# Gated linear attention and two expert layers: warming products, the key-value product and the two highest score levels moved

## The reference

```python
for t in range(S):                      # 4 batches x 8 heads, S = 768, head_dim 48
    state = alpha[:, :, t, :, None] * state + np.einsum('bhd,bhe->bhde', k[:, :, t], v[:, :, t])
    y[:, :, t] = np.einsum('bhd,bhde->bhe', q[:, :, t], state)
...
for e in range(E):                      # x is y as 3072 x 384; 4 experts of 384 x 1024 x 384
    h = np.maximum(x @ w1[e], 0.0)
    out += p[:, e:e + 1] * (h @ w2[e])  # p: domain_probs, normalised over the experts
...
h = x @ w_in                            # 384 x 2048 x 384
g = h * np.clip(h + 3.0, 0.0, 6.0) / 6.0
return g @ w_out
```

## Time and profile before

| | |
|---|---|
| time, median of 3 runs | 1378.64 us (1376.93 to 1380.78) |
| time of the profiled execution | 1379.01 us |
| its span | 1377.2 us |
| PE busy | 1356.5 us, 98% of the span |
| POOL, DVE, ACT busy | 57%, 49%, 39% |
| mean granted clock of TensorE | 0.98 of full |
| end of the prologue (first hidden product) | 70.68 us |

### The profile page before, as it was taken

How to read it: one execution, slowest core, us unless ns; L and a number is a source line. 1 busy time by engine, 2 the same in 40 slices (tenths; PEclk the granted TensorE clock), 3 DMA queues, 4 the chain that set the end, 5 groups by cost and what they waited for, 6 DMA issues and landing times.

```text
span 1377.2 us, 34014 instructions
## 1 busy us (share of the span) xinstructions
PE 1356.5 (98%) x13568; PEld 1107.3 (80%) x13568; DVE 678.3 (49%) x1397; ACT 534.8 (39%) x992; POOL 781.8 (57%) x865
## 2 busy tenths in 40 slices
PE   6899999999999999999999999999999999999998
PEld 5688888888888888888888888888888888888887
DVE  8776665444454544454544454454445343333333
ACT  2233333333354333354433345433335433335543
POOL 8866666655555665565656555656564444444442
PEclk6599999999999999999999999999999999999999
DMA  4243333333333433333433333343322232332331
GB/s 148 82 144 119 118 118 103 121 109 110 97 106 115 140 104 116 106 99 114 134 119 109 105 99 123 104 140 98 113 85 92 93 134 100 107 96 93 101 117 35
DMA packets 69899, 150.33 MB, mean 109 GB/s; under 512 B 8816, under 2 KB 21360, under 8 KB 69744
## 3 DMA queue, kind: packets, MB, share of 16 engines
q1 hardware_dynamic: 69744, 148.16, 34.3%
HBM read 143.36 MB, written 4.77 MB: 108 GB/s over the span
## 4 chain that ended last, share of the span: by engine, by line
PE 97%; POOL 1%; DVE 1%; issue 1%; ACT 0%; DMA 0%; DVEq 0%; POOLq 0%
PE psum L526 43%; PE psum L510 43%; PE psum L426 5%; PE psum L447 1%; PE psum L467 1%; PE psum L482 1%; PE psum L437 1%; PE psum L490 1%; POOL k_lev L906 0%; DMA alpha_q<-qa 0%; POOL decay L869 0%; DVE q_lev L595 0%; DVE psum L637 0%; POOL w_lo L925 0%; ACT x_hi L796 0%
## 5 line engine op out<-in xcount | busy, mean ns | idle before, releaser
L925 POOL TENSOR_TENSOR w_lo<-w_raw,w_hi 128x768 fp32r<-128x768 f32 (+1 forms) x291 | 531.4, 1826 | 541.8 <-ACT w_hi L815 541.8
L809 ACT ACTIVATE h_hi<-psum 128x512 fp32r<-128x512 f32 x288 | 172.3, 598 | 628.0 <-DVE psum L651 553.3
L526 PE MATMUL psum<-h_hi,w_hi 128*128 128x512 f32 x864 | 344.8, 399 | 0.2 <-DVE x_lo L673 0.2
L526 PE MATMUL psum<-h_hi,w_lo 128*128 128x512 f32 x864 | 337.2, 390 | 0.0
L526 PE MATMUL psum<-h_lo,w_hi 128*128 128x512 f32 x864 | 336.7, 390 | 0.0
L510 PE MATMUL psum<-x_hi,w_hi 128*128 128x512 f32 x864 | 336.4, 389 | 0.0
L510 PE MATMUL psum<-x_lo,w_hi 128*128 128x512 f32 x864 | 336.1, 389 | 0.0
L510 PE MATMUL psum<-x_hi,w_lo 128*128 128x512 f32 x864 | 336.0, 389 | 0.0
L651 DVE SCALAR_TENSOR_TENSOR psum<-psum,probs 128x512 f32<-128x512 f32 x192 | 134.2, 699 | 351.3 <-PE psum L510 351.2
L815 ACT ACTIVATE w_hi<-w_raw 128x768 fp32r<-128x768 f32 x288 | 241.5, 838 | 0.0
L663 DVE TENSOR_TENSOR h_lo<-psum,h_hi 128x512 fp32r<-128x512 f32 x288 | 197.7, 686 | 60.9 <-ACT h_hi L809 60.9
(11 more groups left out here) (57 smaller groups left out, 805.8 us busy)
## 6 DMA issues: line engine op xcount, KB each, us to landing
w_raw<-w SPq DMA_DIRECT2D x288, 384.0 KB, 3.1
alpha_q<-qa SPq DMA_DIRECT2D x48, 256.0 KB, 3.5
k_raw<-kk SPq DMA_DIRECT2D x48, 128.0 KB, 3.6
probs<-prob_scratch SPq DMA_DIRECT2D x24, 256.0 KB, 3.8
v_sb<-v SPq DMA_DIRECT2D x48, 96.0 KB, 2.8
out<-result SPq DMA_DIRECT2D x18, 256.0 KB, 3.9
level_sb<-level SPq DMA_DIRECT2D x1, 80.0 KB, 3.1
ident_sb<-ident SPq DMA_DIRECT2D x1, 64.0 KB, 2.8
```

The source lines that it names most:

```text
L526: mm = pe.matmul(out_bank[k], a, x[:, g % DEEP, :], start=first and i == 0, stop=last and i == 2)
L809: act.activation(h_hi[:, g % DEEP, :], h_bank[g % 2][:, :], ACT.Copy).then_inc(hh_made, 1)
L925: op = pool.tensor_tensor(w_lo[:, g % RING, cols], w_raw[:, g % RAW, cols], w_hi[:, g % RING, cols].bitcast(F32), ALU.subtract)
```

## The change

- In the prologue PE's order becomes: score(n+1), one warming product, attend(n), one warming product, turn_k(n+1), one warming product. Two more for each n from 0 to 6; around chunk 7's attend there are five and four as before.
- carry writes both halves into the chunk's own two score banks, with start=False, beside what attend wrote there. Bank 0 is left to turn_k, which now waits for `kn_made` (ACT has copied the keys of the chunk before) in place of `s_made`.
- p_kept exists twice. keep(n) step 0 and the new ACT step wait for attend(n-2) in place of attend(n-1).
- For the chunks 0 to 7, DVE's keep has four steps in place of six. The levels 5 and 4 are copied by ACT in copy_high(n+1), six instructions on 32 or 16 partitions each, placed between odd_k(n+3) and split_x(n). Step 0 becomes a predicated copy, so that it leaves ACT's parts standing, and waits for all six (`high_made`). The zeros around them are written once by POOL at the start, before its first scale_k.

```diff
+def keeps(n):
+    return KEEPS - 2 if n < PER_TILE else KEEPS
...
-        p_kept = sb("p_kept", [P, 2, 2, CH])
+        p_kept = [sb(f"p_kept{i}", [P, 2, 2, CH]) for i in range(2)]
...
 # turn_k
-                need(pe, s_made, carried(n))
+                need(pe, kn_made, carried(n))
...
 # carry
-                            lo = KV_AT + jp * HEAD_D
-                            mm = pe.matmul(kv_bank(n, jj)[own(i), lo:lo + HEAD_D], k_rows[own(jj), jp, own(i)],
-                                           v_sb[n % 2][own(jj), jp, i, :], start=jp == 0 and jj == 0, stop=True,
+                            lo = 512 * jj + KV_AT + jp * HEAD_D
+                            mm = pe.matmul(scores(n)[own(i), lo:lo + HEAD_D], k_rows[own(jj), jp, own(i)],
+                                           v_sb[n % 2][own(jj), jp, i, :], start=False, stop=True,
...
 # PE, prologue
                 keep_warm(1 if n + 1 < PER_TILE else 5)
                 attend(n)
+                keep_warm(1 if n + 1 < PER_TILE else 4)
                 if n + 1 < PER_TILE:
                     turn_k(n + 1)
-                else:
-                    keep_warm(4)
+                    keep_warm(1)
...
 # DVE, keep, step 0
-                    need(dve, y_made, n)
+                    need(dve, y_made, n - 1)
                     dve.wait_ge(p_made, n + 1)
...
+                    if n < PER_TILE:
+                        dve.wait_ge(high_made, HIGHS * (n + 1))
+                        mask = diag_sb[:, :].bitcast(I32).rearrange("p (o r m) -> p o r m", o=1, r=2)
+                        op = dve.copy_predicated(pairs, mask.to_broadcast([P, 4, 2, CH // 2]), both)
+                    else:
+                        mask = diag_sb[:, :].rearrange("p (o r m) -> p o r m", o=1, r=2)
+                        op = dve.tensor_tensor(pairs, both, mask.to_broadcast([P, 4, 2, CH // 2]), ALU.mult)
...
 # ACT
+            def copy_high(n):
...
+                need(act, y_made, n - 1)
+                act.wait_ge(p_made, n + 1)
+                for l in (LEVELS - 1, LEVELS - 2):
+                    x, at = 1 << l, CH // 2 * (l + 1)
+                    for m in range(CH // 2 // x):
+                        for jj in range(2):
+                            rows = slice(64 * jj + 2 * x * m, 64 * jj + 2 * x * m + x)
+                            act.activation(dst[rows, :, (2 * m + 1) * x:(2 * m + 2) * x],
+                                           s[rows, :, at + x * m:at + x * m + x], ACT.Copy).then_inc(high_made, 1)
...
+            copy_high(0)
             for n in range(PER_TILE):
                 copy_k_rows(n)
                 if not first_of_seq(n):
                     decay_state(n)
                 if n + 3 < K_BEFORE:
                     odd_k(n + 3)
+                if n + 1 < PER_TILE:
+                    copy_high(n + 1)
                 split_x(n)
...
 # POOL
+            for i in range(2):
+                pool.memset(p_kept[i][:, :, :, :], 0.0).then_inc(p_zeroed, 1)
```

More of the change, by code:

```diff
@@ L51 @@
 KEEPS = LEVELS
+HIGHS = 6
 K_TOP = PAIRS * CH + CH // 2
@@ L137, in last_of_seq, with kept @@
     return n % SEQ_CH == SEQ_CH - 1
+def keeps(n):
+    return KEEPS - 2 if n < PER_TILE else KEEPS
+def kept(n):
+    return sum(keeps(m) for m in range(n))
 def need(eng, sem, count):
@@ L189, in build @@
         psum = ctx.enter_context(nc.psum_tensor("psum", [P, 8 * BANK], F32))
-        state_bank = psum[:, 0:BANK]
         score_banks = psum[:, BANK:3 * BANK]
@@ L194, in build @@
         h_bank = [psum[:, i * BANK:(i + 1) * BANK] for i in (6, 7)]
-        kt_out = state_bank[:, 0:2 * P]
+        kt_out = psum[:, 0:2 * P]
         in_qa = [sem(f"in_qa{i}") for i in range(QRING)]
@@ L203, in build @@
         in_prob_rows, prob_rows_out, prob_made = sem("in_prob_rows"), sem("prob_rows_out"), sem("prob_made")
-        zeros_made, ones_made = sem("zeros_made"), sem("ones_made")
+        zeros_made, ones_made, p_zeroed = sem("zeros_made"), sem("ones_made"), sem("p_zeroed")
         three_made = sem("three_made")
@@ L210, in build @@
         pv_made, y_made = sem("pv_made"), sem("y_made")
-        keep_made, kn_made, dec_made, s_made = sem("keep_made"), sem("kn_made"), sem("dec_made"), sem("s_made")
+        keep_made, high_made, kn_made, dec_made, s_made = sem("keep_made"), sem("high_made"), sem("kn_made"), sem("dec_made"), sem("s_made")
         yt_made, x_hi_made, x_lo_made = sem("yt_made"), sem("x_hi_made"), sem("x_lo_made")
@@ L264, in scores @@
             return out_banks if n < PER_TILE and n % 2 else score_banks
-        def kv_bank(n, jj):
-            return scores(n)[:, BANK:2 * BANK] if jj else state_bank
         def kv_out(n):
-            stride = (4 if n < PER_TILE and n % 2 else 2) * BANK
-            return psum[:, 0:2 * stride].rearrange("p (a c) -> p a c", a=2)[:, :, KV_AT:KV_AT + 2 * HEAD_D].rearrange(
+            return scores(n)[:, :].rearrange("p (a c) -> p a c", a=2)[:, :, KV_AT:KV_AT + 2 * HEAD_D].rearrange(
                 "p a (b e) -> p b a e", b=2)
@@ L455, in attend @@
                 pe.wait_ge(in_v[n % 2], 16 * (n // 2 + 1))
-                pe.wait_ge(keep_made, KEEPS * (n + 1))
+                pe.wait_ge(keep_made, kept(n + 1))
                 if not last_of_seq(n):
@@ L467, in attend @@
                                 mm = pe.matmul(scores(n)[quarter(jp, x), lo:lo + HEAD_D],
-                                               p_kept[own(jj), i, jp, 32 * th:32 * th + 32],
+                                               p_kept[n % 2][own(jj), i, jp, 32 * th:32 * th + 32],
                                                v_sb[n % 2][own(jj), jp, i, :],
@@ L600, in keep @@
                 s = scores(n)[:, :].rearrange("p (a c) -> p a c", c=SLAB)
-                dst = p_kept[:, :, :, :].rearrange("p i a t -> p (i a) t")
+                dst = p_kept[n % 2][:, :, :, :].rearrange("p i a t -> p (i a) t")
                 if step == 0:
@@ L604, in keep @@
                         dve.wait_ge(in_diag, 16)
-                    need(dve, y_made, n)
+                    need(dve, y_made, n - 1)
                     dve.wait_ge(p_made, n + 1)
                     pairs = dst.rearrange("p a (m r) -> p a r m", r=2)
[L608 to L611, removed]
+                    both = s[:, :, 0:CH].rearrange("p a (r m) -> p a r m", r=2)
+                    if n < PER_TILE:
[5 more added lines that the diff above has]
+                        op = dve.tensor_tensor(pairs, both, mask.to_broadcast([P, 4, 2, CH // 2]), ALU.mult)
+                    op.then_inc(keep_made, 1)
                     return
@@ L615, in keep @@
                     dve.wait_ge(in_mask, 16)
-                dve.wait_ge(keep_made, KEEPS * n + step)
+                dve.wait_ge(keep_made, kept(n) + step)
                 at, x, m = CH // 2 * (l + 1), 1 << l, CH // 2 >> l
@@ L720, in _ @@
                 beside, behind = ((2, 2), (2, 1))[n - PER_TILE + 2] if last else (3, 2)
-                for step in range(KEEPS):
+                for step in range(keeps(n)):
                     keep(n, step)
@@ L774, in odd_k @@
                 act.activation(b, a, ACT.Copy).then_inc(k_odd_made, 1)
+            def copy_high(n):
+                s = scores(n)[:, :].rearrange("p (a c) -> p a c", c=SLAB)
+                dst = p_kept[n % 2][:, :, :, :].rearrange("p i a t -> p (i a) t")
+                if n == 0:
+                    act.wait_ge(p_zeroed, 2)
+                need(act, y_made, n - 1)
[7 more added lines that the diff above has]
+                                           s[rows, :, at + x * m:at + x * m + x], ACT.Copy).then_inc(high_made, 1)
             def copy_k_rows(n):
```

## The result

The changed kernel takes 1373.47 us (median of 5 runs, 1373.37 to 1373.84) where the kernel before takes 1378.76 (1376.93 to 1380.78, 5 runs beside it). The ratio is 0.9961, with a 95% interval from 0.9948 to 0.9973: 5.3 us or 0.4% faster. The forecast was 1370, the range 1366.5 to 1381. That range takes in the time of the kernel before as well, so a time inside it says little by itself; the gain was forecast at 9.2 us and came to 5.3.

The account below looks back on a forecast made before the run. PE at half clock was taken to bound the prologue's chunks. Six spacings from 7.24 to 5.9 (8.0 us), 0.4 in the first chunk and 0.75 in the last make 9.2: 1379.0 to 1369.8, predicted 1370 us, range 1366.5 to 1381.

Parts of the forecast that it names:

- The bound and the main mechanism: Prologue: PE at half clock fills three quarters of a 7.24 us chunk; additional warming products raise the clock.
- The rise: Prologue: clock rises in the first or second chunk running warming product, turn_k, warming product; 2.3 us full-width against 1.87 sufficing.
- The fast chunk: Prologue chunk at full clock, bound by DVE: 5.9 us (5.6 to 6.2) in place of 7.24.
- The 0.2 us added for the meeting of DVE and POOL: Fast chunk: scale_q operations on DVE that ran in POOL's idle time now meet it; 0.2 us added.
- the upper end of 6.2: Fast chunk: reached if the single scale_q step waits up to one POOL operation more, POOL being busy all through.
- The edits costed at nothing: Prologue: turn_k's earlier wait, carry's banks, ACT's six copies (1.5 to 2.0 us, hidden), memsets and second p_kept gain nothing.
- DVE's saving: DVE's keep without two levels: 0.53 us for each chunk, ends 0.33 and 0.63; worth nothing at 1.2 GHz.
- seven chunks fast, none late: Chunks n = 0 to 6 all at full clock, other engines on time: 9.2 us gained; chance 0.40.
- The first hidden product: End of the prologue: it starts at about 61.5 us, with the same 1306.5 us from there on.
- the second rival: Prologue: late rise or one or two clock falls, 2.6 us for each slow chunk; 1372.6 to 1375.2 us, chance 0.21.
- the first rival: Prologue: clock swings with PE's short idles, three or four slow chunks; 1378 to 1380 us, chance 0.22.

Follow-up runs that it names:

- e2: The kernel before with only the two additional warming products for each chunk; 1375.92 us, ratio 0.9972.
- e1: The changed kernel without its two additional warming products for each chunk; 1378.92 us, ratio 0.9993.
- e6: The changed kernel with only the additional warming product ahead of turn_k, none behind it; 1374.26 us, ratio 0.9964.
- e8: The changed kernel with 192 more PE instructions (small products of zeros) in PE's early idle time; 1370.86 us, ratio 0.9936.
- e7: The changed kernel with 64 more PE instructions (small products of zeros) in PE's early idle time; 1372.58 us, ratio 0.9950.
- e9: The changed kernel with 160 more PE instructions (small products of zeros) in PE's early idle time; 1373.23 us, ratio 0.9952.
- e11: The kernel before with 192 more PE instructions (small products of zeros) in PE's early idle time; 1379.59 us, ratio 1.0000.
- e10: The changed kernel with 224 more PE instructions (small products of zeros) in PE's early idle time; 1373.47 us, ratio 0.9950.
- e5: The changed kernel with one further warming product behind turn_k for n = 0 to 6; 1375.60 us, ratio 0.9975.

## Why the prediction was right, and by how much it was off

**The bound and the main mechanism held.** The prologue at half clock was where the time lay, the warming products raised the clock (e2), and the rest of the kernel did not move. e1 shows the condition the other way round: without the clock, nothing.

**The rise came as forecast.** Up from 21.02 us, in the first chunk whose cluster of warming product, turn_k and warming product ran. I had taken two to be needed because of the 1.87 us in the earlier trace rows; e6 shows that one more already suffices.

**The fast chunk was sized well.** 5.9 forecast (5.6 to 6.2), 5.85 measured in the undisturbed chunk of the changed kernel, 5.4 to 5.8 in e8. DVE was the bound in it, with PE hardly behind: the state was taken at 31.10 in a chunk that began at 26.84, 4.26 behind the start where I had 4.1.

```profile
29.21 1.68 DVE L600 TENSOR_TENSOR q_lev<-q_lev,decay 128x256 f32<-128x256 f32 x2
...
31.10 0.35 DVE L641 TENSOR_TENSOR state<-state_decayed,psum 128x192 f32<-128x192 f32 x1
...
31.67 0.40 DVE L600 TENSOR_TENSOR q_lev<-q_lev,decay 128x256 f32<-128x256 f32 x1
32.50 0.61 DVE L597 TENSOR_TENSOR q_lev<-q_lev,decay 128x128 f32<-128x128 f32 x1
```

The 0.2 us added for the meeting of DVE and POOL came near, but not where it was looked for: with POOL busy all through, the single step still took 0.40 us, and the last, smaller one took 0.61 where it takes 0.28 in the kernel before. The chunk stayed well below the upper end of 6.2.

**The edits costed at nothing cost nothing:** turn_k's wait (e1), the copies on ACT (0.25 us each, done 3 us ahead of split_x in the chunk shown), the memsets. DVE's saving was priced at 0.53 with ends of 0.33 and 0.63, and was 0.43 by the instructions and 0.47 by the chunk, since the copy of 256 elements took 0.53 and not 0.44.

**The step that was off is the sum's "seven chunks fast, none late".** It gave 9.2 us, and the two profiled spans differ by 5.7. The first hidden product came at 64.88 us in place of 61.5. The chunks n = 3 and n = 5 took 7.87 and 6.85 us where their neighbours took 5.8: together 3.1 us, nearly all of what was missing; the last piece, n = 6 and 7, had part of its first score at half clock, 2.48 us for 1.6 (in the chain of waits).

The number lies in the band of the second rival, one or two falls of the clock (1372.6 to 1375.2, chance 0.21), but that is partly luck, since the rival had another mechanism: a whole chunk bound by PE at half clock, 2.6 us each. No such chunk came. Most of the loss is the holes' own length. From the score's start to attend's, the chunk n = 3 took 4.40 us where the undisturbed one took 2.56, so 1.8 us more; the rest of it, partly at half clock, took only 0.2 more. The hole in n = 5 is 1.1 us, all that this chunk lost. The two falls together cost about 1.1 us: 0.2 there and 0.9 in the score of 2.48.

The clock didn't swing with each short idle time, as the first rival had it: the chunk from 26.84 to 32.69 has PE busy 4.89 of 5.85 us and the clock at 1.00 to its end and beyond. The Trainium skill tells in "TensorE: Matmul & The Clock Gate" (on a second failure mode) of a kernel whose clock swung with short idles between groups of products. These traces don't agree with it for idles of this kind. Each fall between 22 and 60 us came during a hole of 0.90 us (e7) or more, or soon behind one.

**What was not seen is the holes.** No term of the sum asked whether PE's instructions arrive in time when a chunk of some 370 of them passes in 5.8 instead of 7.2 us. The trace of before had the transfers (110 of them on its page) and no hole from them. In e8, where the clock doesn't fall, the time is 1370.9, within a microsecond of the forecast; in part that is luck too, since its undisturbed chunks, 5.54 and 5.41 us, make up for its holes. In e9, with no fall either but 4.5 us of holes, it is 1373.2.

## What to carry to other kernels

Before taking work off an engine, ask at which clock TensorE runs there: here, at half clock, everything else hid behind it, and dummy products that fill PE's own waits may be the change to make first, after which the other savings begin to count. When a stretch of many small products gets faster, the supply of instructions is a resource like any other: holes put down to "issue" inside a group of equal products, at places a fixed number of instructions apart, are its mark. A few dummy instructions in an idle time move them, which tests the cause and may hide them.

## What the runs showed of the hardware that was not expected

- TensorE stood still for 0.6 to 2.5 us at some of the instruction numbers 193 + 256 k in every kernel whose prologue ran at the higher clock, and at none in the three whose prologue stayed at 0.50 from 22 us on (before, e1, e11). One such hole, 1.17 us in e10, lies where the clock was 0.50.
- A hole was followed by a fall of the clock in one kernel and not in another (0.90 us at 1729 in e7 and 1.35 us at 1473 in e6: a fall; 1.68 us at 1729 in e8: none). Behind a fall the stretches at 0.50 were 3.4 to 13.7 us long.
- The clock record of a trace can begin late: where the changed kernel's shows 1.00 up to 21 us, the lengths of the products say 1.2 GHz. A known product's length is the check.
- One warming product more or fewer for each chunk (e5, e6) changed the spread of single runs more than the median.
